# Scores and outputs of each head on its own 64x64 part of TensorE, and half a weight chunk per step of the first batch

## The reference

```python
# attention: q, k, v are (4, 8, 576, 64); factor 4, scale 1/8
q_d, k_d, v_d = means over 4 neighbouring rows            # 144 rows
out_up = repeat(softmax(scale * q_d @ k_d.T) @ v_d, 4)     # coarse
scores = where(|i - j| < 4, scale * q @ k.T, -1e9)
x = out_up + softmax(scores) @ v                           # coarse + local
x = x.transpose(0, 2, 1, 3).reshape(2304, 512)
h = x @ w_in;   y = (max(h, 0) + alpha * min(h, 0)) @ w_out      # 512 -> 2048 -> 512
h2 = y @ w2_in; out = where(h2 > 0, h2, exp(min(h2, 0)) - 1) @ w2_out
```

## Time and profile before

| | |
|---|---|
| median of 3 runs | 921.67 us (920.73 to 924.37) |
| the profiled execution | 921.41 us, span 919.6 us |
| PE busy | 906.8 us (99% of the span) |
| DVE, ACT, POOL busy | 541.3, 339.1, 281.3 us |
| mean granted TensorE clock | 0.996 of full speed (2.4 GHz) |

### The profile page before, as it was taken

One profiled execution on the slowest core, in us unless ns is written; L12 is line 12 of the kernel. 1 busy time (PEld: TensorE's weight loads), 2 busy tenths in 40 slices (PEclk: granted clock), 3 DMA queues, 4 the chain that ended last, 5 costly groups with the idle time before them and its releaser, 6 DMA issues.

```text
span 919.6 us, 15263 instructions
## 1 busy us (share of the span) xinstructions
PE 906.8 (99%) x5611; PEld 850.2 (92%) x5616; DVE 541.3 (59%) x1071; ACT 339.1 (37%) x784; POOL 281.3 (31%) x399
## 2 busy tenths in 40 slices
PE   8799999999999999999999999999999999999998
PEld 6689999999999999999999998888888888988887
DVE  6665656555655554454455575656865657756563
ACT  6763335334534232241232142323442324423233
POOL 3799882111210145546466541110011100000000
PEclk9999999999999999999999999999999999999999
DMA  7665442222210123544453243444464443634411
GB/s 167 144 159 146 123 123 54 54 54 54 51 44 15 29 64 124 179 131 129 157 198 90 62 145 115 115 117 117 121 183 116 115 121 111 190 117 115 115 47 69
DMA packets 119834, 100.70 MB, mean 109 GB/s; under 512 B 66000, under 2 KB 82384, under 8 KB 119760
## 3 DMA queue, kind: packets, MB, share of 16 engines
q1 hardware_dynamic: 118576, 99.42, 38.3%
q10 hardware_dynamic: 1184, 0.30, 0.2%
HBM read 80.29 MB, written 19.40 MB: 108 GB/s over the span
## 4 chain that ended last, share of the span: by engine, by line
PE 94%; POOL 2%; issue 1%; DVE 1%; DMA 1%; ACT 0%; ACTq 0%; POOLq 0%; DVEq 0%
PE ps L242 29%; PE ps L244 28%; PE ps L243 28%; PE ps L441 3%; PE ps L485 1%; PE ps L423 1%; PE ps L431 1%; PE ps L472 1%; PE ps L456 1%; PE ps L448 1%; DMA qk_nat<-in_k 1%; POOL p_l L702 1%; PE ps L438 0%; POOL p_c L699 0%; POOL w_in_lo L732 0%
## 5 line engine op out<-in xcount | busy, mean ns | idle before, releaser
L244 PE MATMUL ps<-common,w_hi 128*128 128x384 f32 x768 | 258.2, 336 | 0.0
L243 PE MATMUL ps<-common,w_hi 128*128 128x384 f32 x768 | 257.9, 336 | 0.0
L243 PEld LDWEIGHTS ps<-common,w_hi 128*128 128x128 f32 x768 | 144.6, 188 | 0.0
L244 PEld LDWEIGHTS ps<-common,w_hi 128*128 128x128 f32 x768 | 144.3, 188 | 0.0
L242 PE MATMUL ps<-common,w_out_lo 128*128 128x384 f32 x384 | 132.9, 346 | 0.5 <-DVE common L321 0.5
L242 PE MATMUL ps<-common,w_in_lo 128*128 128x384 f32 x384 | 132.7, 345 | 0.0
L317 ACT ACTIVATE common<-act_g 128x384 fp32r<-128x384 f32 x96 | 50.4, 525 | 215.4 <-PE ps L244 125.5
L883 ACT ACTIVATE act_g<-act_g 128x384 f32<-128x384 f32 x96 | 50.5, 526 | 195.1 <-DVE act_g L879 195.1
L242 PE MATMUL ps<-w_hi,common 128*128 128x512 f32 x288 | 113.6, 394 | 0.0
L244 PE MATMUL ps<-w_hi,common 128*128 128x512 f32 x288 | 113.5, 394 | 0.0
L243 PE MATMUL ps<-w_out_lo,common 128*128 128x512 f32 x288 | 113.5, 394 | 0.0
(11 more groups left out here) (104 smaller groups left out, 1533.3 us busy)
## 6 DMA issues: line engine op xcount, KB each, us to landing
ring<-w_in_parts SPq DMA_DIRECT2D x168, 256.0 KB, 2.7
w_in_parts<-parts SPq DMA_DIRECT2D x8, 1280.0 KB, 5.7
qk_nat<-in_q SPq DMA_DIRECT2D x32, 144.0 KB, 2.8
v_nat<-in_v SPq DMA_DIRECT2D x16, 288.0 KB
out<-xT SPq DMA_DIRECT2D x18, 256.0 KB, 2.3
qk_nat<-in_k SPq DMA_DIRECT2D x30, 144.0 KB, 3.1
v_win<-in_v SPq DMA_DIRECT2D x64, 67.5 KB
xT<-in_moe_w_in SPq DMA_DIRECT2D x16, 256.0 KB, 3.2
```

Source lines behind the costliest of these rows:

```text
L243: pe.matmul(psum, l_hi, r_lo, start=False, stop=False)
L244: return pe.matmul(psum, l_hi, r_hi, start=False, stop=stop)
```

## The change

`QM` goes from 96 to 112 rows of scores: head 0 in partitions 0 to 47 (up to 63 filled), head 1 in 64 to 111. `qT` and `qd` are unpadded, with the heads on their own 64 partitions; each score matmul becomes two, one for each head, of 64 rows by 48 or 64 columns in its own quarter of the array. The local output becomes 24 matmuls (6 windows, 2 sides, 2 heads) of 54 key rows, 64 columns and 48 moving columns, all of them in job O1, in the four quarters in turn; side 0 goes to the bank of O0 and side 1 to that of O1. Transposes of the weights are 112 wide. The copies of q and of `pT_l` are one instruction for two, `place_qd` and most zero fills are gone, and the scale of the pooled q sits in the exponential. DVE adds in two blocks of 288 columns instead of three of 192, and waits for the whole output before its coarse copy. POOL splits half a chunk per step of the first batch (two chunks, not four, by its end) and four chunks (2 to 5) in step 4; `w_split` still counts whole chunks. SP loads two chunks ahead instead of one.

```diff
-    COARSE_SCALE = 1.0 / FACTOR ** 2
+    COARSE_SCALE = SCALE / FACTOR ** 2
...
-    QM = HEADS * QW
-    DQ = QW // FACTOR
-    CW = QM // (HEADS * DQ)
-    CB = NW // CW
+    HR = P // HEADS
+    QM = HR + QW
+    CB = SD // QW
...
-            qT, kT = sb("qT", [P, NW, HEADS, QW]), sb("kT", [P, S])
-            qdT, kdT = sb("qdT", [P, NW, HEADS, DQ]), sb("kdT", [P, SD])
-            qd = sb("qd", [P, SD])
+            qT, kT = sb("qT", [P, S]), sb("kT", [P, S])
+            qd, kdT = sb("qd", [P, SD + HR - QW]), sb("kdT", [P, SD])
             p_c, p_l = sb("p_c", [QM, CB, SD]), sb("p_l", [QM, NW, KP])
-            pT_c, pT_l = sb("pT_c", [SC, 2, NW, HEADS, DQ]), sb("pT_l", [2 * KP, NWH, 2, HEADS, QW])
+            pT_c, pT_l = sb("pT_c", [SC, 2, HEADS, SD]), sb("pT_l", [2 * KP, NWH, HEADS, QW])
...
             def score_coarse(pe, u, bank):
-                pe.wait_ge(qd_placed, u + 1)
+                pe.wait_ge(q_pooled, 2 * u + 2)
                 pe.wait_ge(k_pooled, 2 * u + 2)
                 for b in range(CB):
-                    last = pe.matmul(scores_c(bank)[:, b, :],
-                                     qdT[:, CW * b:CW * (b + 1), :, :].rearrange("p w h i -> p (w h i)"), kdT[:, :],
-                                     start=True, stop=True)
+                    for h in range(HEADS):
+                        rows = tile_rows(h)
+                        last = pe.matmul(ps[rows, bank, SD * b:SD * (b + 1)],
+                                         qd[head_rows(h), QW * b:QW * b + rows.stop - rows.start], kdT[head_rows(h), :],
+                                         start=True, stop=True)
                 last.then_inc(sc_done, 1)
             def score_local(pe, u, g, bank):
                 pe.wait_ge(r_copied, 4 * u + 4)
-                pe.matmul(ps[0:QM, bank, 0:GW * KW], twice[:, :, :].rearrange("p h q -> p (h q)"),
-                          mask[:, g:g + GW, :].rearrange("p w k -> p (w k)"), start=True, stop=False)
+                for h in range(HEADS):
+                    rows = tile_rows(h)
+                    pe.matmul(ps[rows, bank, 0:GW * KW], one[head_rows(h, QW), 0:rows.stop - rows.start],
+                              mask[head_rows(h, QW), g:g + GW, :].rearrange("p w k -> p (w k)"), start=True, stop=False)
                 for i, w in enumerate(SLOT_WINDOW[slots(g)]):
-                    last = pe.matmul(scores_l(bank)[:, i, :], qT[:, w, :, :].rearrange("p h q -> p (h q)"),
-                                     kT[:, KEY0[w]:KEY0[w] + KW], start=False, stop=i == GW - 1)
+                    for h in range(HEADS):
+                        last = pe.matmul(ps[head_rows(h, QW), bank, KW * i:KW * (i + 1)],
+                                         qT[head_rows(h), QW * w:QW * (w + 1)],
+                                         kT[head_rows(h), KEY0[w]:KEY0[w] + KW], start=False, stop=i == GW - 1)
                 last.then_inc(sl_done, 1)
...
             def output_coarse(pe, u, bank):
                 pe.wait_ge(vd_done, u + 1)
                 pe.wait_ge(ptc_copied, 2 * u + 2)
                 for x in range(2):
                     for h in range(HEADS):
-                        pe.matmul(ps[D * h:D * (h + 1), bank, 0:SD], vd[:, h, x, :], pT_c[:, x, :, h, :], start=x == 0,
-                                  stop=x == 1)
-            def output_blocks(pe, u, n, bank):
-                if n == 0:
-                    pe.wait_ge(v_win_loaded, V_LOADS * (u + 1))
-                    pe.wait_ge(ptl_copied, 2 * u + 2)
-                for j in range(NBH):
-                    if block_at(j)[0] == n:
-                        for i in (2 * j, 2 * j + 1):
-                            for h in range(HEADS):
-                                to = ps[D * h:D * (h + 1), bank, block_at(j)[1]:block_at(j)[1] + 2 * XW]\
-                                    .rearrange("p (s q) -> p s q", s=2)[:, :, QW * (i % 2):QW * (i % 2 + 1)]
-                                last = pe.matmul(to, v_win[:, i, h, :], pT_l[:, i, :, h, :], start=True, stop=True)
+                        last = pe.matmul(ps[head_rows(h), bank, 0:SD], vd[:, h, x, :], pT_c[:, x, h, :], start=x == 0,
+                                         stop=x == 1)
+                last.then_inc(o_done, 1)
+            def output_local(pe, u):
+                pe.wait_ge(v_win_loaded, V_LOADS * (u + 1))
+                pe.wait_ge(ptl_copied, 2 * u + 2)
+                for i in range(NWH):
+                    for side in range(2):
+                        for h in range(HEADS):
+                            keys = slice(KP * side, KP * side + KW)
+                            at = first_col(side) + QW * i
+                            last = pe.matmul(ps[head_rows(h), bank_of("O", side, u), at:at + QW], v_win[keys, i, h, :],
+                                             pT_l[keys, i, h, :], start=True, stop=True)
...
-                if n == 0:
-                    for h in range(HEADS):
-                        rows = slice(D * h, D * (h + 1))
-                        last = act.activation(qT[rows, per // QW * c:per // QW * (c + 1), h, :],
-                                              ps[rows, bank, 0:per].rearrange("p (w q) -> p w q", q=QW),
-                                              ACT.Copy, scale=SCALE)
-                else:
-                    last = act.activation(kT[:, per * c:per * (c + 1)], ps[:, bank, 0:per], ACT.Copy)
-                last.then_inc(r_copied, 1)
-            def place_qd(act, u):
-                act.wait_ge(q_pooled, 2 * u + 2)
-                if u:
-                    act.wait_ge(sc_done, u)
-                for h in range(HEADS):
-                    rows = slice(D * h, D * (h + 1))
-                    last = act.activation(qdT[rows, :, h, :], qd[rows, :].rearrange("p (w i) -> p w i", w=NW), ACT.Copy,
-                                          scale=SCALE)
-                last.then_inc(qd_placed, 1)
+                act.activation((kT if n else qT)[:, per * c:per * (c + 1)], ps[:, bank, 0:per], ACT.Copy,
+                               scale=1.0 if n else SCALE).then_inc(r_copied, 1)
...
-                for side in range(2):
-                    rows = slice(KP * side, KP * (side + 1))
-                    last = act.activation(pT_l[rows, GP * g:GP * (g + 1), side, :, :].rearrange("p i h q -> p i (h q)"),
-                                          ps[rows, bank_of("TL", g, u), 0:GP * QM].rearrange("p (i q) -> p i q", i=GP),
-                                          ACT.Copy)
-                last.then_inc(ptl_copied, 1)
+                act.activation(pT_l[:, GP * g:GP * (g + 1), :, :],
+                               ps[:, bank_of("TL", g, u), 0:GP * P].rearrange("p (i h q) -> p i h q", i=GP, h=HEADS)
+                               [:, :, :, 0:QW], ACT.Copy).then_inc(ptl_copied, 1)
...
             def copy_coarse(dve, u):
-                dve.wait_ge(o_done, 2 * u + 1)
+                dve.wait_ge(o_done, 2 * u + 2)
...
+                dve.tensor_tensor(
+                    xT[:, b * NXB + nb * side:b * NXB + nb * (side + 1), pair, :].rearrange("p w (i f) -> p w i f", f=FACTOR),
+                    ps[:, bank_of("O", side, u), at:at + HALF].rearrange("p (w i f) -> p w i f", w=nb, f=FACTOR),
+                    coarse_o[:, SD // 2 * side:SD // 2 * (side + 1)].rearrange("p (w i o) -> p w i o", w=nb, o=1)
+                    .to_broadcast([P, nb, XW // FACTOR, FACTOR]), ALU.add).then_inc(x_done, 1)
...
-            LATE = [range(BATCH_UNITS, BATCH_UNITS + 2),
-                    *(range(n, min(n + 4, FC)) for n in range(BATCH_UNITS + 2, FC, 4))]
-            assert len(LATE) == BATCH_UNITS and LATE[-1].stop == FC
+            EARLY = BATCH_UNITS // 2
+            LATE = [range(n, min(n + 4, FC)) for n in range(EARLY, FC, 4)]
+            assert len(LATE) == BATCH_UNITS
...
-            def hi_of_weights(gp, c):
+            def split_weights(gp, c, which):
                 gp.wait_ge(w_loaded[c % WS], 32 * (c // WS + 1))
-                for which in range(2):
-                    last = gp.tensor_scalar(w_hi[:, which, c, :], w_stage[:, c % WS, which, :], 1.0, 0.0, ALU.mult, ALU.add)
-                last.then_inc(w_hi_done, 1)
-            def lo_of_weights(gp, c):
-                gp.wait_ge(w_hi_done, c + 1)
-                for which in range(2):
-                    for cols in (slice(0, DM // 2), slice(DM // 2, DM)):
-                        last = gp.tensor_tensor((w_out_lo if which else w_in_lo)[:, c, cols], w_stage[:, c % WS, which, cols],
-                                                w_hi[:, which, c, cols].bitcast(F32), ALU.subtract)
-                last.then_inc(w_split, 1)
+                gp.tensor_scalar(w_hi[:, which, c, :], w_stage[:, c % WS, which, :], 1.0, 0.0, ALU.mult, ALU.add)\
+                    .then_inc(w_hi_done, 1)
+                gp.wait_ge(w_hi_done, 2 * c + which + 1)
+                for cols in (slice(0, DM // 2), slice(DM // 2, DM)):
```

(50 more changed lines are left out.)

65 lines of the change are left out of this document (27 added, 38 removed).

## The result

The changed kernel takes 925.14 us (median of 8 runs, 924.42 to 927.69) beside 920.31 for the kernel before on the same chips: ratio 1.0057, interval 1.0036 to 1.0078. It is slower by 0.6%; the profiled execution's span is 923.4 us, 3.8 above the 919.6 of the kernel before. The runs of one kernel spread with the mean granted clock: those of the kernel before that stand beside e1 to e4 lie between 918.5 us at 1.0 and 926.3 at 0.991, so differences of a few us are read from the traces too. In `after.py`, FFN matmuls are L239 to L241, scores L438, L447 and L451, transposes L427, L459 and L467, outputs L482 and L494, filler L1041.

A forecast was written before the change was run, and what follows sets the result against it. A ring of short operations was taken to bound the first batch, PE everything from tile 0 on. Terms -4.4 + 5.9 + 1.7 + 3.3 - 0.5 = +6.0 gave 927.5 us, 0.6% slower; 8-in-10 range 916 to 937.

The forecast's parts named there:

- The wait at tile 0: Beginning of tile 0: PE waits for POOL's second half of chunk 1, +5.9 us (+5 to +7).
- The first batch: Before tile 0: shorter steps from faster local scores and one copy of q for two, -4.4 us (-1.9 to -6.5).
- Score pairs: Local scores: two matmuls of 48 weight columns take 50 ns a pair (45 to 80), -8.4 us from tile 0 on.
- Rounds of four: Local output: 48 matmuls in 12 rounds of 100 ns (40 to 160), +2.5 us in 12 units.
- Changes of layout: Scores and outputs from tile 0 on: PE pays for new changes of array layout, +6.7 us.
- PE's time from tile 0 on: Scores, outputs, transposes, masks and layout changes from tile 0 on: +3.3 us in sum (-13.4 to +20.7).
- Elsewhere: Between tiles 0 and 1: PE's 0.53 us wait for DVE goes with two ACT copies, -0.5 us (0 to -0.9).
- POOL's slack: First batch: POOL, idle 0.40 us before the tightest normalisation, does not set the pace, so its halved chunk gains nothing.
- A: Rival: quarters do not overlap, 80 ns a score pair and 160 an output round, 947.5 us; chance 0.10.
- B: Rival: all four quarters overlap fully and changing the layout costs nothing, 911.4 us; chance 0.13.
- C: Rival: the halved chunks do no harm at the beginning of tile 0, 7.6 us less, 920; chance 0.17.
- D: Rival: a second wait, for unit 5's normalisation with 2.2 us to spare, stalls PE by about 2, 930 us; chance 0.10.

The follow-up runs named there:

- e1: The changed kernel with the weight schedule of the kernel before (whole chunks in the first batch, loads one chunk ahead): 914.38 us, 0.9933 of the kernel before.
- e4: The changed kernel, where POOL splits both halves of chunk 1 in step 2 and nothing in step 3: 920.56 us, 1.0006 of the kernel before.
- e2: The kernel before with only the changed weight schedule (half a chunk per step, four in step 4, loads two ahead): 934.83 us, ratio 1.0148.
- e3: The changed kernel, where SP loads the v windows of a step before the late chunk: 921.92 us, 1.0010 of the kernel before.
- e6: e5 with the second half of the coarse output between the two sides of the local one: 925.44 us, 5.5 above e5.
- e7: e1, where a local score group takes its six windows of head 0, then those of head 1: 924.67 us, 10.3 above e1.
- e5: e1, where the local output takes all windows of the second side, then all of the first: 919.96 us, 5.6 above e1.
- e8: e1 with six filler matmuls instead of one behind the local output of steps 0 to 2: 912.14 us, 0.9898 of the kernel before.

## Why the prediction was right

The time (927.5 said, 925.14 measured) and the sign were right, the main cause was right, and that the number came so near is luck. The sum was made of one term that was exact, some that held, and two errors of opposite sign.

- *The wait at tile 0*: 5.9 said, 5.77 measured, released by POOL's last half of chunk 1; e2 shows it without the new layout, e4 takes it away. Slow clock behind it: 1.7 said. Nine matmuls at 0.32 us for 0.17 and the first transposes make about 1.8.
- *The first batch*: -4.4 said; tile 0 began 0.4 early, which with the wait of 4.1 is -4.5, and -3.9 in e3, which has no such wait. The prediction kept the two slow stretches of the kernel before; the changed kernel and e3 have three (mean clock of the first 58 us 0.91 for 0.94). The step from 14.06 to 22.90, without slow clock, was 8.84 for a forecast of 8.9.
- *A wait missed*, 4.1 us. The prediction went through SP's new order for step 3 only. Step 1 has the same order: chunk 2's load waits for chunk 0, which the halving finishes a step later, and the v windows of unit 2 stand behind it. The step that failed is the one that looked for who waits behind a moved load; I did it for one of the two late loads.
- *Score pairs*: 50 ns said, 46 measured, the lower bound. *Rounds of four*: 100 said, the middle of 40 and 160, and 59 measured. Local outputs were to grow by 0.21 us a unit and shrank by 0.25. This is the mis-sized term: 0.46 in 12 units is 5.5 us. The reason I gave for 50 in the pairs (nothing shows both sides small and slow) held for the rounds as well, and I did not use it there. By its own terms the lower end of that sum is -13.0, not -13.4.
- *Changes of layout*: 0.10 in, 0.14 out, 0.12 inside. In L482 to L494 the changed kernel pays 0.10 more (0.64 for 0.54). Into L438 PE takes 0.27 us (91.56 to 91.83), 0.10 over the usual, as said. e6 puts a pair, to 128 rows and back, at 0.47: in that place my 0.12 each was half of it.
- *PE's time from tile 0 on*: +3.3 said, with the -0.5 of "Elsewhere" +2.8. From the outputs of unit 4 to those of unit 15 it was -4.0, in which the 0.53 of the earlier trace rows is contained; it went, as said. PE waits 0.54 and 0.60 for DVE at 71.77 and 73.13, in the lead burst of unit 5's scores (0.32 at 65.22 in the kernel before), which I had not looked at.
- *POOL's slack*: the prediction read the 0.40 us before the normalisation of 45.44 as room that POOL has. It has none there. DVE's L622 takes 0.27 us in that step, 0.17 in the others, and ends with POOL's last split:

```profile
43.63 1.41 POOL L732 TENSOR_TENSOR w_out_lo<-xT,w_hi 128x256 fp32r<-128x256 f32 x2
...
44.81 0.27 DVE L622 TENSOR_SCALAR stats<-stats 96x15 f32<-96x15 f32 x1
```

The wait missed (+4.1) and PE's time taken as dearer than it is (6 to 7 too much) largely cancel. The sign needs both waits: without the one that was forecast the kernel is level with the one before (e4, 1.0006), and without the one that was missed it is level as well (e3, 1.0010). From the events that the prediction knew, 0.6% slower did not follow.

The rivals: A is refuted by the 46 and 59 ns themselves; e7 builds its situation for the scores (41 ns each) and pays 10.3 us. B was right that the pairs overlap fully, and near it for the rounds (59 for 40), but a change of layout has a price: even e1, without either wait, takes 914.4, above B's 911.4. C fell with the 5.77. D did not come in the changed kernel (its normalisation of unit 5 ends at 83.12 and PE asks at 85.86); its wait is the one in e4.

Where neighbours share one part of the array, the pace is that of the weight loads. The Trainium skill ("TensorE: Matmul & The Clock Gate", LDWEIGHTS) gives a weight load as its columns over 1.2 a nanosecond: 80 ns for 96 columns and 40 for 48. The 82 of the earlier trace rows and e7's 41 agree. The floor of about 25 ns between matmul starts in Part 1 of the same page of the Trainium skill, which the prediction quoted, does not hold here: 23 ns in the scores and 15 in the outputs.

## What to carry to other kernels

Small float32 matmuls gain from a quarter of the array each only if neighbours in program order use different quarters; an order that keeps neighbours in one quarter or in the same rows (e5, e7) gives it all back, and in e6 one more change into another group's layout and back costs what ten pairs of score matmuls take. When work is taken off a stage because it might bound it, look first at what that engine does just before the op that closes the stage, and do not take its idle time for slack before you know that the op which releases it was not held up itself (the 0.40 us of the earlier trace rows and of e8). Then look at who needs the result first, and follow every load whose condition moves through its queue, in each step in which it occurs. A change of two parts is worth splitting: one was a gain of 0.7%, the other a loss of twice that.

## What was not expected of the hardware

Four quarters in turn bring matmul starts to 15 ns, with 64-column weight loads among them. In two column halves of the same rows e5's pair takes 51 ns. By the paces of 82 ns for 96 weight columns and 41 for 48 (e7), one load of 64 columns is about 55, an estimate; so the pair costs about one load, not two. And PE's clock is still granted in full from 58 to 60 us, with PE idle since 57.3, and is at half when it comes back at 63. In e1 three slow stretches follow idle times of 1.4 us, one in a step, and six fillers of 512 columns ended them (0.91 to 1.00). The length of the idle time alone does not decide it: in the kernel before PE stands for 1.4 of the 2 us from 35, and no slow stretch follows until 47.

```profile
35.00:37.00 2.00, 0.60 (x6) 0.33 (x5) 1.77 (x8) 1.41 (x5) 1.28 (x2) 1.00 1.16 225
```

And a DVE operation on 15 columns takes 0.17 or 0.18 us in most steps. Begun while POOL splits weights it takes 0.76 and 0.77 in two steps of e8, and ends just behind the split (41.50 for 41.47, and 50.96 for 50.92).
